# A fused convolution and two-layer kernel: prologue reordered, layer 2 ten units behind layer 1 instead of eleven

## What is computed

```
x   : x[s] = sum over k of W[head, k] * x_in[s + k - 6]      (causal, 7 taps)
1   : h = x @ w_in                     (192 -> 2048)
      P = a0 + a1*h + a2*h^2 + a3*h^3
      Q = 1 + |b0|*|h| + |b1|*h^2
      x2 = (P / (Q + 1e-6)) @ w_out    (2048 -> 192)
2   : h = x2 @ w_in2                   (192 -> 2048)
      y = (s * max(h, 0)^2 + b) @ w_out2
```

## Time and profile before

| | |
|---|---|
| median of 3 runs | 1308.73 us (1307.24 to 1309.42) |
| the profiled execution | 1309.7 us, span 1307.9 us |
| mean granted TensorE clock | 0.991 |
| TensorE matmul busy | 1276.3 us, 98% |
| VectorE busy | 1138.5 us, 87% |
| ScalarE busy | 1115.1 us, 85% |
| GpSimd busy | 331.7 us, 25% |
| chain that ended last | TensorE 90%, VectorE 5%, ScalarE 2%, issue 2% |

### The profile page before, as it was taken

How to read it: one execution, slowest core, us unless ns; L and a number is a source line. 1 busy time by engine, 2 the same in 40 slices (tenths; PEclk the granted TensorE clock), 3 DMA queues, 4 the chain that set the end, 5 groups by cost and what they waited for, 6 DMA issues and landing times.

```text
span 1307.9 us, 16349 instructions
## 1 busy us (share of the span) xinstructions
PE 1276.3 (98%) x5984; PEld 1077.7 (82%) x5984; DVE 1138.5 (87%) x1048; ACT 1115.1 (85%) x1072; POOL 331.7 (25%) x147
## 2 busy tenths in 40 slices
PE   5897999999999999999999999999999999999998
PEld 3665888888888888888888888888888888888887
DVE  5998889998999989998899989999899998979830
ACT  5887898888889888889888888998888898888843
POOL 4333222222222222222222222222222222222210
PEclk8998999999999999999999999999999999999999
DMA  5211000010000100001000010001000000000000
GB/s 137 106 33 25 1 1 13 1 37 1 12 0 0 36 0 12 0 0 36 0 12 0 13 23 0 12 0 36 0 12 0 0 12 1 13 1 13 1 13 13
DMA packets 14045, 20.40 MB, mean 16 GB/s; under 512 B 1472, under 2 KB 9664, under 8 KB 13504
## 3 DMA queue, kind: packets, MB, share of 16 engines
q1 hardware_dynamic: 13872, 20.00, 5.4%
q10 hardware_dynamic: 144, 0.01, 0.0%
HBM read 13.72 MB, written 6.29 MB: 15 GB/s over the span
## 4 chain that ended last, share of the span: by engine, by line
PE 90%; DVE 5%; ACT 2%; issue 2%; POOL 1%; DMA 0%; DVEq 0%; SPq 0%; ACTq 0%
PE o L363 25%; PE h L337 9%; PE h L338 9%; PE h L340 9%; PE h L341 9%; PE h L339 9%; PE o_tail L352 4%; PE o L350 4%; PE o_tail L354 4%; PE o L351 4%; PE o L353 4%; DVE work L737 1%; DVE work L704 1%; DVE work L706 1%; DVE work L739 1%
## 5 line engine op out<-in xcount | busy, mean ns | idle before, releaser
L320 POOL TENSOR_TENSOR gl<-work,gh 128x1024 fp32r<-128x1024 f32 x128 | 307.0, 2398 | 896.2 <-ACT gh L566 896.2
L363 PE MATMUL o<-v,work 128*128 128x192 f32 x2048 | 353.3, 326 | 0.0
L363 PEld LDWEIGHTS o<-v,work 128*128 128x128 f32 x2048 | 339.2, 190 | 10.1
L704 DVE SCALAR_TENSOR_TENSOR work<-work,coef,h 128x1024 f32<-128x1024 f32 x128 | 163.7, 1279 | 91.9 <-ACT work L539 91.9
L337 PE MATMUL h<-x_hi,w_hi 128*128 128x512 f32 x512 | 224.4, 438 | 17.6 <-DVE work L709 13.4
L341 PE MATMUL h<-x_tail,w_tail_lo 128*128 128x512 f32 x512 | 205.0, 400 | 0.0
L338 PE MATMUL h<-x_lo,w_hi 128*128 128x512 f32 x512 | 204.6, 400 | 0.0
L340 PE MATMUL h<-x_tail,w_tail_hi 128*128 128x512 f32 x512 | 204.6, 400 | 0.0
L339 PE MATMUL h<-x_hi,w_lo 128*128 128x512 f32 x512 | 204.2, 399 | 0.0
L537 ACT ACTIVATE work<-h,coef 128x1024 f32<-128x1024 f32 x128 | 154.2, 1205 | 27.8 <-PE h L341 21.4
L569 ACT ACTIVATE work<-work 128x1024 f32<-128x1024 f32 x128 | 135.7, 1060 | 42.4 <-DVE work L704 38.8
(11 more groups left out here) (78 smaller groups left out, 1544.8 us busy)
## 6 DMA issues: line engine op xcount, KB each, us to landing
out_dram<-y_out SPq DMA_DIRECT2D x16, 384.0 KB, 2.6
xt<-in_x_main_dram SPq DMA_DIRECT2D x7, 518.0 KB, 4.5
xt_tail<-in_x_tail_dram SPq DMA_DIRECT2D x8, 259.0 KB, 5.1
work<-in_moe_w_out_dram SPq DMA_DIRECT2D x1, 1536.0 KB, 9.7
v<-in_moe_w_out_dram SPq DMA_DIRECT2D x1, 1536.0 KB, 6.3
work<-in_moe_w_in_dram SPq DMA_DIRECT2D x1, 1024.0 KB, 8.4
work<-in_moe_w_in_dram SPq DMA_DIRECT2D x2, 512.0 KB, 5.8
xt<-in_x_main_dram SPq DMA_DIRECT2D x2, 259.0 KB, 6.4
```

The source lines that it names most:

```text
L320: nc.gpsimd.tensor_tensor(gl[:, j % 2, :], r_buf[j % 2], gh[:, j % 2, :].bitcast(F32), ALU.subtract).then_inc(gl_ready, 1)
L363: last = pe.matmul(o2[:, c // 2, c % 2, 0:D], g, v2[:, f, :], start=(f == 0 and c % 2 == 0), stop=(f == FT - 1), skip_group_check=True)
L704: nc.vector.scalar_tensor_tensor(q_buf[buf], w_abs, b0_abs, h_flat, ALU.add, ALU.mult).then_inc(z_done, 1)
```

## The change

- `SKEW` goes from 11 to 10 and `OUT1_LAG` from 3 to 2. Layer 2 follows ten units behind, and S1 handles unit n-2.
- TensorE's order in a step becomes P1(n), S2(m-1), F2(m), S1(n-2). Only at j = 1 behind the last tile does S1 stand first. S1 issues its six matmuls with gh before it waits for gl. F2 is reordered so that a tile's first unit waits for `x2_hi`, `x2_lo` and the tail one after another.
- At j = 2 VectorE's split of `o1` and ScalarE's `x_sum` copy move to the start of the step, ahead of T, W and z.
- Convolution taps on VectorE move to steps 3 to 7 of the even tile and steps 0 and 3 of the odd one, a main and a tail tap in each.
- Prologue: TensorE takes tap 2 of the first tile too, and three taps of the second tile before P1(0). The second tile's input is loaded before `v1`. VectorE's low parts of `v1` wait until GpSimd has made the first quarter of `w1_lo`. ScalarE does T and W of unit 1 before |q| of unit 0, into `num_buf[1]` and `q_buf[1]`, and T and W of unit 2 before |q| of unit 1. GpSimd's weight pieces are 512 columns wide and wait for a count of VectorE's or ScalarE's work (`w_ready`, `g_ready`).
- Weights of layer 2 are loaded in four parts, cast in four casts of 1024 columns (steps 3 to 6) and subtracted in eight pieces of 512 (steps 4 to 11, ahead of gl on GpSimd). The diagonals of the tail get their own place and are made one or two per step from step 6 to 9.

The diff, cut to its core:

```diff
-    SKEW = 11
-    OUT1_LAG = 3
+    SKEW = 10
+    OUT1_LAG = 2
     OUT2_LAG = 1
-    X2_STEP = OUT1_LAG - 1
+    X2_STEP = OUT1_LAG
...
-    TAPS_AT = {(0, 1): (("pair", 0), ("tail", 0)), (0, 4): (("pair", 1),), (0, 5): (("pair", 2), ("tail", 1)),
-               (0, 6): (("pair", 3), ("tail", 2)), (0, 7): (("pair", 4), ("tail", 3)),
-               (1, 0): (("pair", 5), ("tail", 4)), (1, 1): (("pair", 6), ("tail", 5)), (1, 4): (("tail", 6),)}
-    PE_TAPS_OF_FIRST = (3, 4, 5, 6)
-    DVE_TAPS_OF_FIRST = (0, 1, 2)
-    DIAG_ORDER = (3, 4, 5, 6, 0, 1, 2)
-    CONV_AT = {0: (("second", (0, 1)),), 1: (("second", (2, 3)),), 2: (("second", (4, 5, 6)),),
-               4: (("pair_a", (0, 1, 2)),), 5: (("pair_a", (3, 4, 5)),),
-               6: (("pair_a", (6,)), ("pair_b", (0, 1, 2))), 7: (("pair_b", (3, 4, 5, 6)),),
-               9: (("tail", (0, 1, 2)),), 10: (("tail", (3, 4, 5, 6)),)}
+    TAPS_AT = {(0, 3): (("pair", 0), ("tail", 0)), (0, 4): (("pair", 1), ("tail", 1)), (0, 5): (("pair", 2), ("tail", 2)),
+               (0, 6): (("pair", 3), ("tail", 3)), (0, 7): (("pair", 4), ("tail", 4)),
+               (1, 0): (("pair", 5), ("tail", 5)), (1, 3): (("pair", 6), ("tail", 6))}
+    PE_TAPS_OF_FIRST = (2, 3, 4, 5, 6)
+    DVE_TAPS_OF_FIRST = (0, 1)
+    TAPS_BEFORE_UNITS = (0, 1, 2)
+    CONV_AT = {0: (("second", (3, 4)),), 1: (("second", (5, 6)),),
+               4: (("pair_a", (0, 1, 2)),), 5: (("pair_a", (3, 4, 5, 6)),), 6: (("pair_b", (0, 1, 2)),),
+               7: (("pair_b", (3, 4, 5, 6)),), 8: (("tail", (0, 1, 2)),), 9: (("tail", (3, 4, 5, 6)),)}
...
+        raw_w2 = [work2[:, 0], work2[:, 1]]
+        raw_w2_tail = [work2[:, 2], raw_w1_tail_late[:, :]]
+        tail_diag = [work2[:, 2, k * P:(k + 1) * P] for k in range(TAPS)]
...
+        W2_HIGH_AT = {3: ("tail", 0), 4: ("main", 0), 5: ("main", 1), 6: ("tail", 1)}
+        W2_LOW_AT = {4: ("tail", 0, 0), 5: ("tail", 0, 1), 6: ("main", 0, 0), 7: ("main", 0, 1),
+                     8: ("main", 1, 0), 9: ("main", 1, 1), 10: ("tail", 1, 0), 11: ("tail", 1, 1)}
+        W2_HIGH_COUNT = {("tail", 0): 9, ("main", 0): 10, ("main", 1): 11, ("tail", 1): 12}
+        TAIL_DIAG_AT = {6: (0,), 7: (1, 2), 8: (3, 4), 9: (5, 6)}
...
+            sp.dma_start(xt[:, 1, :], x_main[:, 1, 0:HALO + TOK]).then_inc(x0_second_loaded, 16)
             sp.dma_start(raw_v1, w_out1).then_inc(v1_loaded, 16)
...
+                    sp.wait_ge(v1_lo_ready, 2)
+                    load_w2_tail(0)
+                    for half in range(2):
+                        sp.dma_start(raw_w2[half], w_in2[0:P, W2_HALF[half]]).then_inc(w2_loaded[half], 16)
                     sp.wait_ge(w_lo_ready, 8)
                     sp.dma_start(v2[:, :, :], w_out2).then_inc(v2_loaded, 16)
-                    sp.wait_ge(v1_lo_ready, 2)
-                    sp.dma_start(raw_w2, w_in2[0:P, :]).then_inc(w2_loaded, 16)
+                    sp.wait_ge(w_lo_ready, 10)
+                    load_w2_tail(1)
...
+            pool.wait_ge(w_ready, 1)
             low_of_w1(PIECES[1], 5)
-            low_of_w1(PIECES[2], 7)
+            pool.wait_ge(w_ready, 2)
+            pool.wait_ge(t3_done, 1)
+            for c in LAST_HALVES:
+                low_of_weight(w1_lo[:, c], raw_w1[:, c], w1_hi[:, c], 7)
+            low_of_weight(w1_tail_lo[:, LAST_HALVES[0]], raw_tail(LAST_HALVES[0]), w1_tail_hi[:, LAST_HALVES[0]], 8)
...
+                    if isinstance(n, int) and n in W2_LOW_AT:
+                        rows, half, part = W2_LOW_AT[n]
+                        c = slice(half * (FF // 2) + part * TOK, half * (FF // 2) + (part + 1) * TOK)
+                        from_raw = slice(part * TOK, (part + 1) * TOK)
+                        pool.wait_ge(g_ready, n - 1)
+                        if rows == "main":
+                            low_of_weight(w2_lo[:, c], raw_w2[half][:, from_raw], w2_hi[:, c],
...
+            def second_product_1(n, k, buf):
+                pe.wait_ge(gh_ready, counted(n - OUT1_LAG + 1))
                 for half in range(2):
                     f = 2 * k + half
                     c = slice(half * TOK, (half + 1) * TOK)
-                    first, final = f == 0, f == FT - 1
                     tail = v1_tail[:, f].rearrange("p a b -> p (a b)")
-                    pe.matmul(o1[:, :], v1_hi[:, f, :], gh[:, buf, c], start=first, stop=False)
+                    pe.matmul(o1[:, :], v1_hi[:, f, :], gh[:, buf, c], start=(f == 0), stop=False)
                     pe.matmul(o1[:, :], v1_lo[:, f, :], gh[:, buf, c], start=False, stop=False)
-                    pe.matmul(o1_tail[:, :], tail, gh[:, buf, c], start=first, stop=False)
-                    pe.matmul(o1[:, :], v1_hi[:, f, :], gl[:, buf, c], start=False, stop=final)
-                    last = pe.matmul(o1_tail[:, :], tail, gl[:, buf, c], start=False, stop=final)
+                    pe.matmul(o1_tail[:, :], tail, gh[:, buf, c], start=(f == 0), stop=False)
+                pe.wait_ge(gl_ready, counted(n - OUT1_LAG + 1))
+                for half in range(2):
+                    f = 2 * k + half
+                    c = slice(half * TOK, (half + 1) * TOK)
+                    tail = v1_tail[:, f].rearrange("p a b -> p (a b)")
+                    pe.matmul(o1[:, :], v1_hi[:, f, :], gl[:, buf, c], start=False, stop=(f == FT - 1))
+                    last = pe.matmul(o1_tail[:, :], tail, gl[:, buf, c], start=False, stop=(f == FT - 1))
                 last.then_inc(out1_done, 1)
+            def first_product_of_layer_2(k, x2p, t2):
...
+                if k == 0:
+                    pe.wait_ge(x2_hi_ready, counted(t2 + 1))
+                for half in range(2):
+                    pe.matmul(h2[:, half, :], w2_hi[:, c[half]], x2_hi[x2p][:, :], start=True, stop=False)
+                    pe.matmul(h2[:, half, :], w2_lo[:, c[half]], x2_hi[x2p][:, :], start=False, stop=False)
+                if k == 0:
+                    pe.wait_ge(x2_lo_ready, counted(t2 + 1))
+                for half in range(2):
+                    pe.matmul(h2[:, half, :], w2_hi[:, c[half]], x2_lo[x2p][:, :], start=False, stop=False)
+                if k == 0:
+                    pe.wait_ge(x2_tail_hi_ready, counted(t2 + 1))
+                    pe.wait_ge(x2_tail_lo_ready, counted(t2 + 1))
+                for half in range(2):
+                    pe.matmul(h2[:, half, :], w2_tail_hi[:, c[half]], x2_tail[x2p][:, :], start=False, stop=False)
+                    last = pe.matmul(h2[:, half, :], w2_tail_lo[:, c[half]], x2_tail[x2p][:, :], start=False, stop=True)
+                last.then_inc(h2_ready, 1)
...
+            conv_taps(1, xt[:, 1, :], TAPS_BEFORE_UNITS, 0, TAPS - 1)
...
+                    if unit(n - OUT1_LAG) and not tile(t) and j == OUT1_LAG - 1:
+                        second_product_of_layer_1(n, j, t)
                     if tile(t):
...
+                        first_product_of_layer_2(k2, x2p, t2)
                     if not tile(t):
                         second_product_of_layer_2(t, j, m, k2)
+                    if unit(n - OUT1_LAG) and (tile(t) or j != OUT1_LAG - 1):
+                        second_product_of_layer_1(n, j, t)
...
+                    if j == X2_STEP and tile(t - 1):
+                        act.wait_ge(out1_done, counted(t * UNITS))
+                        act.wait_ge(x2_tail_lo_ready, counted(t - 1))
+                        nc.scalar.copy(x2_sum, o1_tail[TAIL:P, :]).then_inc(x2_tmp_ready, 1)
...
+                        high_of_w1_main(2)
+                        high_of_w1_tail(2)
+                        first_steps(1, h2_flat, num_buf[1], q_buf[1])
+                    if first(t) and j == 1:
+                        act.wait_ge(t3_done, 1)
+                        act.wait_ge(r0_ready, 1)
+                        first_steps(2, h1_flat, t_buf, w_abs)
...
+            dve.wait_ge(w_lo_ready, 4)
...
+                    if j == X2_STEP and tile(t - 1):
+                        split_o1(t, hi, lo)
+                        sum_o1_tail(t)
+                        split_o1_tail(t, tail)
...
-                    if j == X2_STEP and tile(t - 1):
-                        split_o1(t, hi, lo)
-                        sum_o1_tail(t)
-                        split_o1_tail(t, tail)
```

More of the change, by code:

```diff
@@ L164, in conv_rational_relu2_kernel @@
         w1t_loaded = [sem(f"w1t_loaded{piece}") for piece in range(3)]
-        w2_loaded, w2t_loaded, v2_loaded = sem("w2_loaded"), sem("w2t_loaded"), sem("v2_loaded")
+        w2_loaded = [sem(f"w2_loaded{half}") for half in range(2)]
+        w2t_loaded = [sem(f"w2t_loaded{half}") for half in range(2)]
+        v2_loaded = sem("v2_loaded")
         y_stored = sem("y_stored")
@@ L202, in in_h2, with is_unit_1, ahead @@
             return isinstance(n, int) and n < SKEW and n % 2 == 1
+        def is_unit_1(n):
+            return isinstance(n, int) and n == 1
+        def ahead(n):
+            return isinstance(n, int) and n in (1, 2)
         def unit(n):
@@ L316, in phase @@
```

(55 more changed lines are left out.)

120 lines of the change are left out of this document (57 added, 63 removed).

## The result

The changed kernel takes **1321.87 us** (median of 4 runs, 1320.41 to 1322.17) against 1309.03 us for the kernel before in the same comparison: ratio 1.0104, 95% interval 1.0091 to 1.0116. That is slower by 1%, outside the range of 1293 to 1316, where I had forecast 1305.7. The profiled execution took 1321.9 us, its span grew from 1307.9 to 1320.1 us.

A forecast was written before the change was run, and what follows sets the result against it. TensorE's issue order was taken to bound the middle, VectorE's chain the prologue. Prologue -16.8, middle +9.3, end +3.8 and clock +0.7 gave -3.0 us: 1306.7 profiled, forecast 1305.7 by the median, range 1293 to 1316 (own range 1300 to 1312).

The forecast's parts named there:

- z(10) after 7.42 + 3.21: 101.6: Prologue: z(10) starts at 101.6 us, one VectorE step of 7.42 and the split's 3.21 after z(9) at 91.0.
- + 0.3 per diagonal: Prologue, z(3) to z(9): 0.3 us added to ScalarE's step for each diagonal it makes.
- the prologue's working: Start of the kernel: step-by-step times up to P1(12) at 115.7, ending 118.0; 16.8 us gained, bounds 11 and 18.
- P1(0) at full clock, z(0) at 22.0: Prologue: P1(0) near 17.0 at full clock, h after 2.5 instead of 4.7 us; z(0) at 22.0, before 24.46.
- their terms: Prologue, z(3) to z(9): steps of 7.9, 7.8, 9.65, 8.3, 7.4 and 7.8 us, 48.9 in all.
- The collision of gl(0) with e(1): Prologue: gl(0) is late on ScalarE's account and runs into e(1), about 1.4 us.
- The middle: P1(13) to P1(127): 11.4 for square late at S2, 1.2 for late gl, less 3.3: +9.3 us, bounds 0 to 17.
- The end: Behind P1(127): S1(127), now first, waits for gh and gl, ending at +22.9 instead of +19.1: +3.8 us, bounds 2 and 6.
- The 0.7 us for the clock: End: a 2.6 us pause may drop TensorE to 1.2 GHz; 0.7 us added, a third of 2.2.
- Rival A: Middle: square comes in time, the 0.8 us at j=2 shrinks to 0.15; total -12.3, 1296.4 us; chance 0.18.
- Rival B: Middle: the pause at S2 drops TensorE's clock for a block per tile; +31, 1336.5 us; chance 0.10.
- Rival C: Prologue, units 4 to 9: gl ends late behind weight pieces, e takes 3.05 instead of 1.28; +9, 1314.7 us; chance 0.17.

The follow-up runs named there:

- e2: Changed kernel, each tail-tap group waiting only for its own diagonals, the seven tail diagonals made in steps 6 to 8: 1311.29 us, ratio 1.0028.
- e8: e2 plus F2 ahead of S2 in every step but j=2, plus GpSimd's gl(8) waiting for the split as in e6: 1300.34 us, ratio 0.9943.
- the first attempt, e4: Changed kernel with, behind the last tile, S1 last in its step and S2 ahead of F2 at j=0, 1 and 2: 1323.16 us, ratio 1.0110.
- the second gained 0.3%: e8 with S1(127) last in its step (1298.56 us), then also S2(119) ahead of F2(120) one step later: 1296.81 us, ratio 0.9912.
- e6: e2 with GpSimd's gl(8) in step 10 waiting until VectorE's split of the first tile is done: 1309.84 us, ratio 1.0012.
- e1: Changed kernel, each tail-tap group waiting only for its own diagonals instead of all 14: 1314.32 us, ratio 1.0049.

## Why the prediction was wrong

**The step that failed** is in the prologue: "z(10) after 7.42 + 3.21: 101.6". I priced the diagonals on the engine that makes them ("+ 0.3 per diagonal") and put the wait for them at nothing, since I never asked who waits. The wait for a count of 14 stands unchanged in the code that issues the tail taps, now one step ahead of where the table makes the last two. TensorE stood there for 13.3 us, and by e2 it cost the kernel 10. Behind it lay a second error of 2 us, the clash of gl(8) and the split, which shows only once the wait is gone. With both out, z(10) starts at 102.03 and P1(12) at 116.16: the rest of the prologue's working was right to half a us, and the gain there is 17.1 us by P1(12) (its end at 118.5 against 135.59), where I had put 16.8.

Point by point, in the order of the prediction:

- **P1(0) at full clock, z(0) at 22.0**: right. P1(0) starts at 17.24, its second half 1.25 us later, five matmuls at 0.25; z(0) at 22.28. z(3) 42.34 (42.0), z(9) 91.37 (91.0), and the six steps between them are each within 0.13 us of their terms. The collision of gl(0) with e(1) is there, at 1.26 us more than usual (priced 1.4):

```profile
37.30 2.54 DVE L841 SCALAR_TENSOR_TENSOR work<-work,coef 128x1024 f32<-128x1024 f32 x1
```

- **The middle** was right in mechanism, and 2.0 us too small. The losses behind the split and behind gl come to 7 x 0.85 + 7 x 1.0 = 13.0 us, where 11.4 + 1.2 = 12.6 stood: 0.4 us. A usual step takes 9.585 instead of 9.572 (410.13 to 419.71, 439.73 to 449.32 and the like), over 115 steps some 1.5 us. ("Fourteen tiles x 0.8 = 11.4" was not exact: the product is 11.2, or 11.5 with the 0.82 of the offsets.) The steps of e8 have it too, so it doesn't come from S2 standing ahead of F2; what it comes from stays open.
- **The end**: S1(127) finds gh and gl late, as forecast, at 1264.20 and 1266.65, and ends 23.0 behind P1(127) (forecast 22.9). The 0.7 us for the clock did not come: the granted clock was 1.00 from 1262 to 1268. But the pause in front of it was 1.44 us and not the 2.6 that I had worked out, as TensorE came to S1(127) later, in part for a wait of 0.81 for the relu before F2 that I had not looked for. That wait costs nothing more, since S1(127) ends by gl either way. In the place of the 0.7 stands a wait of 0.8 for the split's tail, where ScalarE's `x_sum` copy came behind relu and square. 4.9 against 4.5 is so near by luck: a term that did not come and a wait that I had not seen are of one size.
- **Rival A** (square in time): no, 14 waits. **Rival B** (clock): no; the granted clock was 1.00 in the middle, with a loss of 0.85 to 1.0 us in each tile. The Trainium skill (TensorE: Matmul & The Clock Gate, A second HAM failure mode) tells of a kernel whose clock oscillates by frequent short idles between groups of matmuls; at the size and spacing of idle time in this middle it did not happen. **Rival C** (the prologue by GpSimd's gl beside e) had the sign and the place, but not the mechanism: of units 4 to 9 no e was long, while the split of step 10, which I had costed at its later 3.21, was hit in e2.

The range failed because all three rivals were ways in which my steps could be mis-sized, and none was that a wait in the unchanged code now comes ahead of what it waits for.

## What to carry to other kernels

When work is moved to a later step, list each wait in the code, unchanged ones too, that counts this work, and check for what count it waits and at which step: a wait for "all of them" ties the first consumer to the last producer, and costs nothing only as long as all are made ahead. When an in-order engine gets a new order, the due time of every input moves; the same work in the order P1, F2, S2, S1 (in all steps but j=2) cost 9 us less than as P1, S2, F2, S1, since the latest input went to the latest consumer. At the end of a pipeline the steps get short and inputs late, so its order has to be worked out step by step: the first attempt here moved the waits, the second gained 0.3%.

## What the runs showed of the hardware

- Two overlapping operations that read SBUF with both inputs, one on VectorE and one on GpSimd, took the time of one after the other: 0.69 us became 2.73 (e2, undone in e6). It was a small operation of 64x512 that paid, for the length of a large one that had started 0.15 us ahead of it. In e6, z(10), which reads h, ran at its usual 1.28 us beside the same gl(8).
- A wait of 1.90 us of TensorE was followed by a granted clock of 0.64 over the next 4 us (e4); waits of 1.44 and 0.8 us, 2.4 us apart, left it at 1.00 (the kernel after). Waits of 2.85 and 2.24 us, 4.5 us apart, were followed by 0.60 from 104 to 108 (e2), one of 4.88 us by 0.53 from 96 to 100 (e1). In the prologue of the kernel after, where TensorE stood for 13.3 us, it was 0.72 from 96.6 to 104 and 1.00 from 104 on.
